# Stage 0 of a fused delta-rule attention and two feed-forward layers: its own step order on six PSUM banks, and the columns of group 1 placed anew

## The reference, cut to what matters

```python
for t in range(S):                       # S = 768, batch 4, 8 heads, head_dim 48
    y[t] = q[t] @ state
    v_old = state^T k_n[t]               # k_n = k / (norm(k) + 1e-6)
    state += beta[t] * outer(k_n[t], v[t] - v_old)
x = y as (3072 tokens, 384)
h = relu(x @ w_in)                       # 384 x 2048
x = (h * h) @ w_out                      # 2048 x 384
gate = sigmoid(x @ w_gate)               # 384 x 1536
y = (gate * (x @ w_val)) @ w_last        # 1536 x 384
```

## Time and profile before

| what | value |
|---|---|
| median of three runs | 1008.27 us |
| profiled execution, its own time | 1009.32 us |
| span of the profiled execution | 1007.5 us |
| granted TensorE clock, mean | 0.976 of full speed |
| TensorE (PE) busy | 960.3 us, 95% |
| VectorE (DVE) busy | 543.4 us, 54% |
| ScalarE (ACT) busy | 481.4 us, 48% |
| GpSimd (POOL) busy | 13.2 us, 1% |
| first matmul of `hidden` | at 95.13 us |

### The profile page before, as it was taken

The page is one execution under the profiler, slowest core; times in us unless marked ns, Lnnn a source line. Parts: engine busy times, 40 slices in busy tenths (PEclk is TensorE's granted clock), DMA queues, the critical chain, the costliest instruction groups (busy, mean ns, idle before and its releaser), DMA issues.

```text
span 1007.5 us, 23481 instructions
## 1 busy us (share of the span) xinstructions
PE 960.3 (95%) x10030; PEld 491.6 (49%) x10030; DVE 543.4 (54%) x1075; ACT 481.4 (48%) x865; POOL 13.2 (1%) x27
## 2 busy tenths in 40 slices
PE   2876999999999999999999999999999999999998
PEld 1464565465456456546544444444444444444443
DVE  6978957957866885794326542432422422423322
ACT  4874575666576477556659832132222222222221
POOL 0000000000000000000000000000000000000000
PEclk7867999999999999999999999999999999999999
DMA  9515015015004202201124010010100100100000
GB/s 310 122 35 127 2 34 126 35 35 127 32 4 97 62 34 62 67 33 36 62 92 159 1 63 1 0 62 0 41 21 0 62 0 0 62 0 0 31 0 31
DMA packets 20996, 52.16 MB, mean 52 GB/s; under 512 B 2672, under 2 KB 12912, under 8 KB 20528
## 3 DMA queue, kind: packets, MB, share of 16 engines
q1 hardware_dynamic: 20320, 50.60, 17.8%
q10 hardware_dynamic: 592, 0.33, 0.2%
HBM read 41.48 MB, written 9.44 MB: 51 GB/s over the span
## 4 chain that ended last, share of the span: by engine, by line
PE 88%; DVE 5%; issue 2%; ACT 2%; DMA 1%; SPq 0%; POOL 0%; DVEq 0%; POOLq 0%
PE psum L642 75%; PE psum L556 3%; PE psum L487 1%; PE psum L513 1%; DMA raw_a<-in_w_in 1%; PE psum L543 1%; PE psum L500 1%; PE psum L571 1%; PE psum L525 1%; ACT w L825 1%; PE psum L585 1%; DVE work L1130 1%; PE psum L452 1%; DVE attn L1089 1%; ACT w L731 1%
## 5 line engine op out<-in xcount | busy, mean ns | idle before, releaser
L642 PE MATMUL psum<-work,attn 128*128 128x512 f16 x1944 | 419.9, 379 | 0.1
L642 PE MATMUL psum<-work,w 128*128 128x512 f16 x1728 | 386.3, 380 | 9.7 <-issue 5.9
L642 PEld LDWEIGHTS psum<-work,attn 128*128 128x128 f16 x1944 | 190.2, 98 | 229.7 <-DVE work L1130 0.6
L642 PEld LDWEIGHTS psum<-work,w 128*128 128x128 f16 x1728 | 164.3, 98 | 204.5 <-issue 9.5
L731 ACT ACTIVATE work<-work 128x512 f16<-128x512 f32 (+1 forms) x264 | 155.7, 624 | 143.3 <-DVE work L1263 140.2
L1263 DVE SCALAR_TENSOR_TENSOR work<-psum,work 128x512 f32<-128x512 f32 x72 | 49.8, 692 | 273.0 <-PE psum L642 261.8
L731 ACT ACTIVATE work<-psum,scal 128x512 f32<-128x512 f32 x90 | 60.5, 687 | 169.6 <-PE psum L642 169.5
L1111 DVE SCALAR_TENSOR_TENSOR work<-work 128x512 f16<-128x512 f16 x96 | 66.1, 690 | 61.6 <-ACT work L731 59.8
L731 ACT ACTIVATE attn<-psum 64x384 f32<-64x384 f32 (+5 forms) x160 | 66.0, 442 | 66.2 <-PE psum L513 34.6
L731 ACT ACTIVATE work<-psum 128x512 f32<-128x512 f32 x96 | 57.2, 596 | 64.3 <-PE psum L642 62.9
L1069 DVE TENSOR_TENSOR attn<-attn 128x31 f32<-128x31 f32 (+15 forms) x186 | 63.7, 343 | 6.4
(11 more groups left out here) (97 smaller groups left out, 558.7 us busy)
## 6 DMA issues: line engine op xcount, KB each, us to landing
attn<-in_kt SPq DMA_DIRECT2D x24, 192.0 KB, 4.3
attn<-in_v SPq DMA_DIRECT2D x24, 192.0 KB, 4.5
attn<-in_kn SPq DMA_DIRECT2D x24, 192.0 KB, 3.8
x_spill<-work SPq DMA_DIRECT2D x6, 768.0 KB, 3.4
xt<-x_spill SPq DMA_DIRECT2D x6, 768.0 KB, 5.1
attn<-in_qt SPq DMA_DIRECT2D x20, 192.0 KB, 4.2
y_out<-work SPq DMA_DIRECT2D x5, 768.0 KB, 3.6
work<-in_w_out SPq DMA_DIRECT2D x1, 3072.0 KB, 24.3
```

The lines of the kernel that those rows point to most:

```text
L642: m = mm(dst, x, z, start=first and i == 0, stop=last and i == len(a) - 1)
```

## The change

- Stage 0 gets an order of its own: OTHER[0] moves nearly every fill to an earlier step, solves both chunks' `mid` and `off` one after the other instead of deferring them, and ends the chain at step 18 instead of 31. Banks of fills in stage 0 (except kk of group 1) are the least recently used of six (5, 6, 7, 2, 3, 4) instead of three in turn. The first fills other than kk in banks 2, 3, 4 (qk of chunk 0, both halves, and mid 0) wait for all 12 weight pieces (PIECE_SHARED).
- The bank of a fill and the step of its reading come apart: READ_LATER has qk of chunk 1 read at step 12 (filled at 9) and off 1 read at step 9 (filled at 7).
- The keys of group 1 are loaded ahead of v, q and kn of group 0. Their products (kk of group 1) are made at steps 0 and 1, between the weight pieces. The 12 weight pieces go in fours to steps OPEN, 0 and 1 over the banks 1, 3, 4, 2.
- w_out's parts: high at steps 1, 9, 9, 10, small at 9, 12, 19, 19, low at 7, 11, 13, 19. The last small parts and the last low part come behind the split of the activations. The first `hidden_act` and the first `rest_of_hidden` wait for them.
- ScalarE makes x_hi of group 0 (`first_high_parts`). The maximum is taken by chunk (`max_of_chunk`), chunk 0 at step 13. `place_e` of group 0 is done in two halves at steps 3 and 8.
- `keep_clock` behind fills instead of ahead: 4 after mid 0, 1 after mid 1, and for chunk 1 4 after dr, 2 after su, 14 after xt.
- `column_steps` for group 1 uses the steps of stage 0 only between `start` (13) and `xsplit` (18). What the tables then say: column 0 at step 15 of stage 0. In stage 1: columns 1 to 4 at step 0, 5 to 8 at 1, 9 and 10 at 2, 11 and 12 at 3, 13 to 15 at 4, 16 and 17 at 5, 18 at 6, 19 and 20 at 7, 21 to 23 at 8, 24 to 26 at 9, 27 to 30 at 10.

```diff
 NB = 3
+NB_FIRST = 6
 STEPS = 2 * (N1 + LAG)
...
 OTHER = {
-    0: dict(mid=(2, 2), off=(8, 15), qk=(7, 19), ks=(-7, 14), dr=(13, 20), grow=(14, 25), xt=(14, 28), xmax=28, xscale=31, xsplit=31, kk=(0, 0), lanes=5, norm=6, start=8, small=(3, 7, 17, 17), hi_out=(0, 4, 8, 9), first_out=(7, 8, 19, 21)),
+    0: dict(kk=(0, 1), qk=(2, 9), mid=(3, 5), off=(4, 7), dr=(6, 13), grow=(8, 14), ks=(-7, 10), xt=(11, 15), lanes=3,
+            norm=3, root=7, xmax=16, xscale=17, xsplit=18, start=13, place_e=(3, 8), hi_out=(1, 9, 9, 10), small=(9, 12, 19, 19),
+            first_out=(7, 11, 13, 19), first_max=13),
     1: dict(rows=11, scale_v=13, mid=(14, 15), off=(16, 23), qk=(6, 12), ks=(16, 24), dr=(17, 25), grow=(18, 26), xt=(19, 26), xmax=27, xscale=29, xsplit=31, kk=(9, 15), lanes=17, norm=18, start=18),
...
     return order
+READ_LATER = {("qk", 0, 1, 0): 12, ("qk", 0, 1, 1): 12, ("off", 0, 0, 1): 9}
 FILLS = {}
 FILL_AT = {}
+READ_AT = {}
+PIECE_SHARED = set()
+_last, _filled = [-1] * NB_FIRST, [0] * NB_FIRST
 for _s, _step, *_fill in sorted((f for s in range(GROUPS) for f in fills_of(s)), key=lambda f: f[0:2]):
-    FILLS[tuple(_fill)] = len(FILLS)
-    FILL_AT.setdefault((_s, _step), []).append(tuple(_fill))
+    _fill = tuple(_fill)
+    _kind, _g = _fill[0:2]
+    _n = NB_FIRST if _s == 0 and (_kind, _g) != ("kk", 1) else NB
+    _b = min(range(_n), key=lambda b: _last[b])
+    _last[_b] = len(FILLS)
+    _filled[_b] += 1
+    if _b >= NB and _kind != "kk" and _b not in {FILLS[f][0] for f in PIECE_SHARED}:
+        PIECE_SHARED.add(_fill)
+    FILLS[_fill] = (_b, _filled[_b])
+    FILL_AT.setdefault((_s, _step), []).append(_fill)
+    READ_AT.setdefault((_s, READ_LATER.get(_fill, _step)), []).append(_fill)
 def bank_of(f):
-    return FILLS[f] % NB
+    return FILLS[f][0]
 def count_of(f):
-    return FILLS[f] // NB + 1
+    return FILLS[f][1]
 EVACUATION = {"qk": 1.4, "ks": 0.6, "su": 1.1}
...
     start, end = place(g - 1, "start") + 1, place(g, "rows")
-    steps = [(g - 1, step) for step in range(start, STEPS)]
+    steps = [(g - 1, step) for step in range(start, STEPS if g > 1 else place(0, "xsplit"))]
     steps += [(g, step) for step in range(0, end)]
...
 SCALE_COLUMNS = (7, 22)
-REST_BANK, REST_PIECES = (2, 3, 4, 1, 5, 6, 7, 2, 3, 4, 1, 2), 12
-REST_FIRST = 12
+REST_PIECES = 12
+REST_BANK = (1, 3, 4, 2) * 3
+REST_AT = {OPEN: (0, 1, 2, 3), 0: (4, 5, 6, 7), 1: (8, 9, 10, 11)}
 WARM_START = 11
-WARM_AHEAD = ("mid", "off", "qk", "ks", "dr")
+WARM_BEHIND = {("mid", 0, 0): 4, ("mid", 1, 1): 1, ("dr", 1, 1): 4, ("su", 1, 1): 2, ("xt", 1, 1): 14}
 def delta_rule_ffn_kernel(nc, kt, qt, kn, v, beta, mask, ident, w_in, w_out, w_gate, w_val, w_last, y):
...
             sp.dma_start(raw_o.rearrange("p (k f) -> p k f", k=N1), w_out.rearrange("(k p) f -> p k f", p=P)).then_inc(in_w["wo"], 16)
+            for c in range(NC):
+                load_k(1, c)
             load_v(0)
             load_kn(0)
-            for c in range(NC):
-                load_k(1, c)
             for s in range(GROUPS - 1):
...
             def open_fill(*f):
+                if f in PIECE_SHARED:
+                    pe.wait_ge(w_lo_done, REST_PIECES)
                 if count_of(f) > 1:
...
                 open_fill("kk", g, c, x)
-                if g == 1:
-                    pe.wait_ge(w_lo_done, 7)
...
                 for kind, g, c, x in FILL_AT.get((s, step), []):
-                    if s == 0 and step > OPEN and kind in WARM_AHEAD and x == 0:
-                        keep_clock(1)
...
                         turn(g, c, x)
+                    if s == 0:
+                        keep_clock(WARM_BEHIND.get((kind, c if kind not in ("mid", "off") else x, x), 0) if g == 0 else 0)
...
                         pe.wait_ge(w_out_done, W_PIECES)
+                        for b in range(NB, NB_FIRST):
+                            pe.wait_ge(bank_read[b], max(n for a, n in FILLS.values() if a == b))
...
                     attention(s, step)
-                    if s == 0 and step == OPEN:
-                        for n in range(REST_FIRST):
-                            rest_of_first(n)
-                    for n in range(REST_FIRST, REST_PIECES):
-                        if s == 0 and step == place(0, "rest")[n - REST_FIRST]:
+                    if s == 0:
+                        for n in REST_AT.get(step, ()):
                             rest_of_first(n)
...
                 elif kind == "off":
-                    if x == 0:
-                        act.wait_ge(e_placed, g + 1)
+                    if g == 0 or x == 0:
+                        act.wait_ge(e_placed, NC * g + NC if g else x + 1)
...
                 n = N1 * m + k
+                if n == 0:
+                    act.wait_ge(w_small_done, W_PIECES)
+                    act.wait_ge(w_out_done, W_PIECES)
                 act.wait_ge(h_full, n + 1)
...
                 run(w1h[:, 4 * part:5 * part][:, at], raw_o[:, at], scale=cell(SMALL_W)).then_inc(w_small_done, 1)
+            def first_high_parts():
+                act.wait_ge(x_scaled, 5)
+                act.wait_ge(w_small_done, 1)
+                act.wait_ge(w_out_done, 1)
+                for kc in range(KC):
+                    run(x_hi[:, kc], xt32[:, TOK * kc:TOK * (kc + 1)], scale=cell(X + 2)).then_inc(x_cut, 1)
...
             def rest_of_hidden(k, m):
+                if (k, m) == (0, 0):
+                    dve.wait_ge(w_out_done, W_PIECES)
...
                 V.tensor_reduce(cell(X), xt32[:], AX.X, ALU.max, apply_absolute_value=True).then_inc(part, 1)
+            def max_of_chunk(c):
+                for x in range(2):
+                    wait_taken(dve, "xt", 0, c, x)
+                link(V.tensor_reduce(scal[:, 32 + KC * c:32 + KC * (c + 1)],
+                                     xt32[:].rearrange("p (k c f) -> p k c f", k=KC, c=NC)[:, :, c], AX.X, ALU.max,
+                                     apply_absolute_value=True), xmax_first, c + 1)
...
                     x = xt32[:, TOK * kc:TOK * (kc + 1)]
-                    V.tensor_scalar(x_hi[:, kc], x, cell(X + 2), None, ALU.mult).then_inc(x_cut, 1)
+                    if n > 0:
+                        V.tensor_scalar(x_hi[:, kc], x, cell(X + 2), None, ALU.mult).then_inc(x_cut, 1)
...
                             weight_scale(SCALE_COLUMNS.index(j), (WI, WO)[SCALE_COLUMNS.index(j)])
+                            if j == SCALE_COLUMNS[1]:
+                                V.tensor_scalar(cell(SMALL_W), cell(WO + 2), 1.0 / LO_GAIN, None, ALU.mult).then_inc(small_scaled, 1)
...
-                    for f in FILL_AT.get((s, step), []):
+                    for f in READ_AT.get((s, step), []):
                         evacuate(*f)
+                    if s == 0 and step == place(0, "first_max"):
+                        max_of_chunk(0)
                     if chain and step == place(s, "xmax"):
                         for x in range(2):
                             wait_taken(dve, "xt", s, NC - 1, x)
-                        x_partial_max(xmax_part)
+                        if s == 0:
+                            max_of_chunk(1)
+                            V.tensor_reduce(cell(X), scal[:, 32:32 + NC * KC], AX.X, ALU.max).then_inc(xmax_part, 1)
+                        else:
+                            x_partial_max(xmax_part)
                     for n in range(W_PIECES):
                         if s == 0 and step == place(0, "first_out")[n]:
```

More of the change, by code:

```diff
@@ L116, in other_work @@
 def other_work(s, step):
-    us = sum(EVACUATION.get(kind, 0.0) for kind, *_ in FILL_AT.get((s, step), []))
+    us = sum(EVACUATION.get(kind, 0.0) for kind, *_ in READ_AT.get((s, step), []))
     for name, cost in (("rows", 4.3), ("scale_v", 3.2), ("xmax", 1.8), ("xscale", 1.0), ("xsplit", 4.0), ("lanes", 2.2),
@@ L182, in delta_rule_ffn_kernel @@
         o_bank = [psum[:, b, :] for b in (2, 3, 4)]
-        a_bank = [psum[:, b, :] for b in (5, 6, 7)]
+        a_bank = [psum[:, b, :] for b in (5, 6, 7, 2, 3, 4)]
         v_bank = [psum[:, b, :] for b in (5, 6)]
@@ L276, in delta_rule_ffn_kernel @@
         zeroed = sem("zeroed")
-        bank_full = [sem(f"bank_full{b}") for b in range(NB)]
-        bank_read = [sem(f"bank_read{b}") for b in range(NB)]
+        bank_full = [sem(f"bank_full{b}") for b in range(NB_FIRST)]
+        bank_read = [sem(f"bank_read{b}") for b in range(NB_FIRST)]
         lanes_cleared = sem("lanes_cleared")
@@ L282, in delta_rule_ffn_kernel @@
         lane_step = sem("lane_step")
+        xmax_first = sem("xmax_first")
         lower_placed, lower_placed_first = sem("lower_placed"), sem("lower_placed_first")
@@ L741, in place_e @@
                     rows = slice(BL * q, BL * (q + 1))
-                    last = run(e_s[rows, :, 0:BL], e_s[rows, :, BL:CH])
-                last.then_inc(e_placed, 1)
+                    last = run(e_s[rows, units, 0:BL], e_s[rows, units, BL:CH])
+                last.then_inc(e_placed, n)
             def evacuate(kind, g, c, x):
```

(19 more changed lines are left out.)

6 lines of the change are left out of this document (3 added, 3 removed).

## The result

| | before | after |
|---|---|---|
| median | 1008.95 us of 7 | **1011.79 us** of 7 |
| lowest to highest | 1006.84 to 1010.36 | 1011.30 to 1013.43 |
| profiled execution, own time | 1009.32 | 1013.43 |
| its first `hidden` | 95.13 | 92.78 |
| its end of `rest_of_hidden(5)` | 124.3 | 129.75 |

The ratio is 1.0033, with a 95% interval from 1.0023 to 1.0042. The change costs 2.8 us. The prediction was 1007.3 us with a range up to 1010.5, so it is wrong, and on the side of the slow rival. The profiled execution of after is the longest of its seven, 1.6 us over the median. Single executions of one kernel differ by that much here, so a comparison of two profiles shows where time goes, and only the medians say how much.

A forecast was written before the change was run, and what follows sets the result against it. Stage 0 was taken as bound by a TensorE, ScalarE and VectorE relay, stage 1 by TensorE. Of 7.5 us gained, 1.0 was left: 1009.32 - 1.0 = 1008.3, less 1.05 to the median, 1007.3; range 1003.5 to 1010.5.

The forecast's parts named there:

- the slow rival: Stage 0: clock falls at the gap before qk of chunk 1, returns only at the end; 5.0 more, 1012.3; chance 0.15.
- The start of stage 0, worth nothing: Stage 0 up to the transposes at 45.02: a fourth bank gains nothing, one moved scalar instruction adds 0.2 us.
- The give-back in stage 1: VectorE in stage 1 gets columns 1 to 10 (7.1 us) and more; `rest_of_hidden(5)` ends at 125.0, later by 0.7.
- The relay: Stage 0's chain between TensorE, ScalarE and VectorE: starts at 49.2, first `hidden` at 87.6, stage 0 ends 7.5 us sooner.
- The weight pieces: Stage 0: 8 pieces and two key fills take 10.6 us, to 48.5; ScalarE's copy then ends at 49.2.
- mid, off and dr of chunk 0: Stage 0, after qk at 51.3: mid done 52.5, off 54.9, dr 57.3; qk of chunk 1 starts at 64.7.
- qk of chunk 1 2.1 and ks 1.0: Stage 0, TensorE: qk of chunk 1 from 64.7 to 66.8, then ks to 67.9.
- Behind ks: Stage 0, after ks: mask to 73.5, dr at half clock 75.5, su 80.8, maximum from 83.6, first `hidden` 87.6.
- `project(5)`: Stage 1, TensorE: it starts at 125.05 instead of 126.56, so 1.5 us of the gain are left.
- ScalarE's 10.7 us: Stage 1, placing e to the keys of group 2: 10.7 instead of 12.0, so ks of group 1 starts at 133.0.
- The faster relay: Stage 0: both qk take 1.1, second dr stays at full clock; stage 0 ends at 84.7, whole 1004.4; chance 0.22.
- The no-give-back rival: Stage 1: VectorE's columns find room and all 7.5 us arrive at the end, 1000.8; chance 0.08.

The follow-up runs named there:

- columns back: The changed kernel with columns 0 to 7 of group 1 done in stage 0, at steps 9 and 14: 1007.25 us, ratio to before 0.998.
- columns alone in the old kernel: The kernel before with only columns 1 to 30 of group 1 moved to stage 1, column 0 at step 9: 1013.52 us, ratio 1.004.
- four banks: The changed kernel with four banks instead of six for the fills of stage 0: 1013.21 us, ratio to before 1.0054.
- the one without `keep_clock`: The changed kernel without its idle matmuls behind mid, dr, su and xt; the 11 at the start stay: 1015.31 us, ratio to before 1.0073.
- gaps filled: The changed kernel with idle matmuls behind group 1's key products (9) and chunk 0's su (10) and transposes (18): 1009.55 us, ratio to before 1.0006.
- the first gap: The changed kernel with only 9 idle matmuls added, behind the first products of keys of group 1: 1011.36 us, ratio to before 1.0027.
- the one more: 13 columns in stage 0 and gaps filled, plus 5 idle matmuls behind chunk 0's first yy and 5 more behind its transposes: 1006.62 us, ratio 0.9982.
- both together: The changed kernel with columns back and gaps filled, both edits: 1006.30 us, ratio to before 0.9975.
- the mask first: Against the one more: w_out's low part behind chunk 1's mask, columns 11 and 12 back in stage 1, 15 idle matmuls behind xt, not 23: 1004.95 us.
- the low part early: The changed kernel with the last low part of w_out on VectorE at step 13 instead of step 19: 1010.27 us, ratio to before 1.0017.

## Why the prediction was wrong

**The start of stage 0, worth nothing.** Right. The transposes start at 44.96 (45.02 before).

**The give-back in stage 1.** Right in its length, and it is the mechanism of the result. From column 1 to the end of `rest_of_hidden(5)` the prediction has 33.7 us, and it took 129.75 - 96.08 = 33.7. TensorE's waits for it were put at 5 to 7 us in stage 1 and were only 3.5, in two. Another 1.7 us went into `project(0)` and the `hidden` behind it, whose 18 matmuls ran at half clock behind the first wait (5.73 us against 4.06 at full clock). Both lie in time that TensorE would have had to wait for the end of VectorE's list anyway. That work added to this list passes on nearly one for one is shown from both sides, by the columns back (-4.5 us) and by the columns alone in the old kernel (+4.6). All this was in the forecast, so it isn't why the time came out longer than predicted.

**The relay: this step failed.** It was to bring the first `hidden` to 87.6 and brought it to 92.78. By its terms:
- *The weight pieces* "end at 49.2". They ended at 50.94. TensorE had stood for 2.42 us before piece 5, and the clock was at 0.50 in 38 to 40 us. Filling that gap took the time back (qk at 49.04), so the cause is shown in the profiles: +1.7. With four banks, where the gap was 1.59 us, the clock stayed up and qk started at 49.15 without any fill.
- *mid, off and dr of chunk 0*: 1.4 more up to qk of chunk 1, half of it the 0.71 inside dr. A gap of 0.4 to 1.0 stands there in every profile of the new order except the one without `keep_clock`. Its cause stays open.
- *qk of chunk 1 2.1 and ks 1.0.* Mostly at half clock (0.60 in 68 to 70, 0.50 in 70 to 72) they took 4.9 us together (67.82 to 72.72): +1.8. This is a piece of the slow rival, which had the fall at this gap.
- Behind ks the lengths were right. From the end of ks to the end of the mask 5.5 (5.6 predicted), dr at half clock 1.96 (2.0), from su to the maximum 3.0 (2.8), from the maximum to the first `hidden` 4.3 (4.0).

The Trainium skill, page TensorE: Matmul & The Clock Gate, Part 1, says that half clock is the default, released by activity, with a phase that varies from run to run. I had used it only for one gap. The trace agrees: the slow stretches stand behind 2.42 and 2.34 us without work in stage 0, and behind 2.13 and 1.40 in stage 1. That the place varies shows at the second yy of chunk 0, slow in one profile (2.33 us) and not in another (1.37).

**`project(5)`.** The prediction has it at 2.05. In the profile of after it took 3.80, with the clock at 0.50, and ks of group 1 followed at 139.01, not at 133.0. Of these 6.0 us the late relay is 4.8 and the slow `project(5)` 1.75, less 0.5 for which ScalarE was predicted to hold ks: from 129.81 to 139.01 TensorE had no gap, so ScalarE's 10.7 us decided nothing. The 1.75 are probably no part of the median. With the columns late, the fall at `project(5)` stands in three profiles of eight (after, gaps filled, no `keep_clock`), and in none of five with columns back. After's profile less this term is 1011.7, beside a median of 1011.79. That is argued from single profiles, not shown. What is left is the relay: 1007.3 and 4.8 less 0.5 make 1011.6. That this meets the median is partly luck. The profile of after gets 0.8 us back at the end of stage 1 (ks of group 1 is 5.0 us later than before, the first `hidden` of stage 2, 173.50 against 169.31, only 4.2), and the median of seven runs of before, 1008.95, is 0.7 above the 1008.27 that the prediction went by. Neither was in the sum, and they nearly cancel.

**The rivals.** The faster relay fell with the first qk, 2.08 at full clock. The no-give-back rival fell by the 3.5 us of new waits in stage 1. The slow rival had the right sign and one of the right places, and 0.5 us too much.

**The range.** I gave the slow rival 0.15 with the argument that it needs the clock to fall before 65 us. It fell before 40 us, at a gap that the prediction itself creates, since the first four pieces and the keys' fill are done by 35.4 and piece 5 waits until ScalarE frees a bank at 37.8. The prediction named the wait and didn't cost the clock behind it. It also treated the 7.5 us as a source that the give-back then takes from, without asking what is left if half of it fails: with a relay gain g the working gives g - 8.2 + 2.2 (8.2 is what `rest_of_hidden(5)` moves back against the first `hidden`, 2.2 the slack at `project(5)`), which is a loss of 3.7 us for g = 2.35. Measured were 2.8.

**What stays open.** The parts of the clock are shown in single profiles, as longer instructions. In the medians they are worth less: 0.4 for the first gap, 2.2 for three, 0.95 on top of the columns back, and a loss for the one more. Only the 2.2 is clear of the noise. Part of that is that a fall moves (the first gap filled). Another part may be that executions of one kernel differ in where it falls: of after, the gaps filled and both together, those with a lower mean clock are mostly the longer ones, but of the columns back, 1005.95 and 1008.85 us have the same 0.981. Which places fall in how many executions, no run here shows.

## What to carry to other kernels

When work is moved off a relay into the stage behind it, add up the list of the engine that gets it, and compare its end with the one consumer that has the least slack: time gained ahead of it comes through only up to that slack. Work that the first stage can hide in its waits is best left there (with 8 columns instead of 1 in stage 0 the whole is 4.5 us shorter, and 13 make the relay no longer than 8). Count waits by stage before using them: the 6.7 us of the whole run held 3.2 that were there before. And before a later or sooner start is put down to an edit, find the place where two profiles part, since a fall of the clock of 1 to 2 us hid or imitated the effect of three edits here. Put a price on the clock behind every gap that a new order opens on TensorE, not only behind the longest.

## What the runs showed of the hardware

- With one gap filled by idle matmuls, the profile has the fall of the clock at the next sparse stretch (yy behind 1.44 us, 2.13 us for 40 records). The gains of filled gaps don't add up here.
- The same five idle matmuls in yy took 1.25 us behind 0.90 us without work in one profile and 2.31 behind 1.45 in another. So filling a gap did not always hold the clock.
- A fill of 64 f32 matmuls of 48 rows took 2.08 us for both halves in stage 0 (qk) and 1.09 in stage 1, at full clock both times. In stage 1 the halves read from different rows.
- The medians of before are steady to 0.25 us (1008.70 to 1008.95 in four sets), while single executions of one kernel spread over 1.6 to 5.6 us (1003.79 to 1005.37 with the mask first, 1008.26 to 1013.87 with the low part early).
- The eight profiles with the columns late all have a wait of 1.4 us ahead of `project(5)`. In three of them it then took 3.5 to 3.8 us, in five 2.1. A gap of the same length, ahead of the same nine matmuls, lost the clock in one profile and kept it in another.
